# Block edges of an attention, MLP and expert kernel: evictions at the end of a slot, staging in a block's first slot, embeddings fetched sooner, and the second tile's rows turned amid products

## The chip, the cores and the metric

The kernel runs on one core of one Trainium2 chip. The metric is the device time of one execution in microseconds. Three executions of the kernel before took 914.99 to 915.56 us, with a median of 915.32 us.

## What is computed

Three stages follow each other, all in float32 at the interface:

```
attention: q, k, v of (4 batches, 8 heads, 576, 64), causal, window of 128, ALiBi bias
mlp:       h = x @ w_in (512 -> 2048);  g = h * clip(h + 3, 0, 6) / 6;  x = g @ w_out     (2304 rows)
router:    logits = norm(x) @ norm(expert_emb).T / tau;  expert = argmax;  gate = softmax at argmax
experts:   out[rows of e] = gate * (relu(x @ w1[e]) @ w2[e])      (8 experts, 512 -> 1024 -> 512)
```

## The kernel before

Every large product is taken in three passes of a rounded type (fp32r): each operand is split in a high part and a low part (the difference), and high by high, low by high and high by low are summed in PSUM. So between two products there is always a pair of small steps: one engine casts the high part, another subtracts it.

**Attention and MLP run interleaved.** Attention is cut in 40 steps (20 groups of query rows by 2 halves of the heads). One iteration `it` of a loop, written once for each engine, holds `scores(it)`, the softmax of it on DVE and ACT, `transposes(it-1)`, `values(it-2)` and `stage(it+1)`, the transposes that bring q and k of the next step in place (`ps_stage`, copied by ACT in `stage_copy`). The MLP is cut in 9 blocks of 256 rows, and each block in 16 slots, one for each 128 columns of its hidden size: slot m has `up(m)` (12 products of 256 columns into `ps_h`, L736) and, two slots later (LAG = 2), `down(m-2)` (6 products of 512 columns into `ps_y`, L751). Between them ACT makes `clip` (L1027), DVE `gated` (L1247), ACT casts `gated_hi` (L1031), and DVE subtracts `gated_lo` (L1250). `slots(it)` says which slots iteration `it` holds, mostly 3 or 4. The first two of an iteration stand before its transposes, the others behind; on ACT the first two stand between the pairs of exponentials. Iteration 14 has one slot alone (31), iteration 15 begins block 2 with slot 32.

**The block edge.** `ps_y`, two banks of block sums, is emptied once a block: ACT copies bank 0 (L1021) and DVE bank 1 (L1243) to `y_sb`. `down` of the next block's first slot waits for both. In the code before, each engine does so at the start of `slot(m)` with f = LAG, that is slot 2 of the next block:

```
def slot(m):
    blk, f = divmod(m, FC)
    if f == LAG and blk:
        act.wait_ge(pe_g, m - LAG)
        ...
        act.copy(y[:, 0, :], ps_y[0][:]).then_inc(ev_y[0], 1)
```

SP then stores the rows (L417). A block's first `up` waits for `x_lo` of the block's last attention step (L1218), which comes behind that step's `values` (L717), ACT's `x_hi` (L1007) and whatever stands ahead of it in DVE's queue. The blocks' edges lie in iterations 10, 15, 19, 23/24, 28, 33, 37 and 41; in 5, 15, 19, 28, 33 and 37 the iteration's first slot is a block's first.

**The router.** For blocks 0 to 6, DVE takes the dot products of the rows with the 8 unit embeddings (`router`, L1229, 16 instructions a block), spread over the slots of the next block. The embeddings are normalised, written to DRAM and read back to all partitions (`en_all`, 2 MB, L481) by SP at iteration EN_AT, after POOL has split all MLP weights, since they share memory with the weights' staging. Within block 1 the router's instructions stand in slots 25 to 31, two or three in each.

**The expert part.** Rows are gathered by POOL in 25 tiles of 128 rows (`fetch`, L592), turned (`turn_x`, L835), multiplied by w1 (`up_high`, `up_low`, L867), passed through a ReLU by ACT (L1125), turned (`turn_h`, L891), copied by ACT as high part and as raw values (`take_hT`, L1140, L1143), subtracted on POOL (`split_h`, L604; `split_x`, L598, for the tile's rows), multiplied by w2 (`expert_down`, L902) into one bank, and evicted by ACT with the gate as scale (`take_rows`, L1134). POOL scatters them (`put`, L613). `expert_down` has 16 products with the high part, then 8 with the low part; an optional `between` stands between these. The first two tiles (AHEAD) are worked before the tables of all tiles are there, in an order written out by hand: down(0), turn_h(1), down(1). DVE splits the expert weights (L1553, L1555); those of the second expert's w2 wait for `split_h(1)`.

Of the kernel before, what the change touches and what calls it, by code (L numbers as in the profile page):

```python
# [54 lines left out]
def _program(nc, q, k, v, w_in, w_out, emb, tau, w1, w2, y_dram, en_dram, out):  # L55
# [22 lines left out]
    STEPS = NG * NQ  # L78
# [23 lines left out]
    LAG = 2  # L102
# [42 lines left out]
    EMB_AT, EN_AT = FIRST + 2, FIRST + 5  # L145
# [27 lines left out]
    with ExitStack() as ctx:  # L173
# [334 lines left out]
        def _(pool):  # L508
# [122 lines left out]
            fetch(2)  # L631
            fetch(3)
            pool.wait_ge(dve_sc, 3)
            put(0)
            split_h(1)
# [16 lines left out]
        def _(pe):  # L652
# [186 lines left out]
            for it in range(LASTK + 1):  # L839
# [3 lines left out]
                if it < STEPS:  # L843
                    scores(it)
                for m in mine[:2]:
                    slot(m)
# [7 lines left out]
                if it + 1 < STEPS and it >= FIRST:  # L854
                    stage(it + 1)
# [39 lines left out]
            def expert_down(t, between=None):  # L895
# [10 lines left out]
                pe.wait_ge(act_hh, HB * (t + 1))  # L906
                for f in range(FCE):
                    if f % FP == 0:
                        wait(pe, w2_split, NC * e + (f // FP + 1))
# [35 lines left out]
            expert_down(0)  # L945
            turn_h(1)
# [16 lines left out]
        def _(act):  # L963
# [46 lines left out]
            def slot(m):  # L1010
                blk, f = divmod(m, FC)
                if f == LAG and blk:
                    act.wait_ge(pe_g, m - LAG)

                    reach(act, st_y, 16 * (blk - 1))
                    reach(act, dve_dot, 2 * E * min(blk - 1, NBLK - 2))
                    if blk == NBLK:
                        act.wait_ge(pe_yT, 2)
                    if blk == 1:
                        act.wait_ge(st_zero, 16)  # L1020
                    act.copy(y[:, 0, :], ps_y[0][:]).then_inc(ev_y[0], 1)  # L1021
# [22 lines left out]
                if 10 <= f <= FC + 1:  # L1044
                    if f == FC + 1:
                        take_xT(0)
                    first_expert(f - 10)

# [66 lines left out]
            slot(SLOTS + LAG)  # L1115
# [33 lines left out]
            relu(1)  # L1149
            take_rows(0)  # L1150
            take_hT(1)
# [15 lines left out]
        def _(dve):  # L1167
# [65 lines left out]
            def slot(m):  # L1233
                blk, f = divmod(m, FC)
                if f == LAG and blk:
                    dve.wait_ge(pe_g, m - LAG)
                    reach(dve, st_y, 16 * (blk - 1))
                    reach(dve, act_sq, 2 * (blk - 1))
                    if blk == NBLK:
                        dve.wait_ge(pe_yT, 2)  # L1240
                    if blk == 1:
                        dve.wait_ge(st_zero, 16)
                    dve.tensor_copy(y[:, 1, :], ps_y[1][:]).then_inc(ev_y[1], 1)  # L1243
# [7 lines left out]
                if 0 < blk < NBLK - 1 and f > LAG:  # L1251

                    late, span = (6, FC - LAG - 7) if blk == 1 else (0, FC - LAG - 1)
# [37 lines left out]
                if f == FC - 3:  # L1291
                    order_of_experts()

# [201 lines left out]
            slot(SLOTS + LAG)  # L1495
# [100 lines left out]
```

## Time and profile before

| | |
|---|---|
| median of 3 executions | 915.32 us |
| the profiled execution | 914.71 us |
| its span, first to last instruction | 912.7 us |
| TensorE busy | 873.6 us, 96% |
| DVE, ACT, POOL busy | 485.1, 430.3, 234.9 us |
| granted TensorE clock, mean | 0.994 |
| first expert product | at 589 us |

The profile is one execution of the program. Its page gives each engine's busy time, the costliest groups of instructions by line, and the idle time just before them with what ended it. The timeline lists instructions in order of time. "PE" is TensorE's products, "PEld" its weight loads. The ends of products are modelled: two that follow each other without a pause overlap in the record. What lies around the span, 2.0 us of the profiled time, is not in the trace.

### The profile page before, as it was taken

The numbers are of one execution on the slowest core, as the hardware profiler recorded it, in microseconds if no ns is written. First come the engines' busy times: TensorE is split into PE (matmuls) and PEld (weight loads), VectorE is DVE, ScalarE is ACT, GpSimd is POOL, SyncE is SP. The second block draws the span as 40 slices with busy tenths as digits, with TensorE's granted clock in tenths as the row PEclk, the third lists the DMA queues.
The fourth block names the chain that finished last, engine by engine and source line by source line (L and its number), as shares of the span: only waits on it lengthen the run. The fifth ranks groups of instructions, "written<-read, shape, count | busy, mean of one in ns | idle before, by whom it ended". The sixth has DMA issues, their size and how long they took to land.

```text
span 912.7 us, 17359 instructions
## 1 busy us (share of the span) xinstructions
PE 873.6 (96%) x5796; PEld 744.1 (82%) x5796; DVE 485.1 (53%) x1421; ACT 430.3 (47%) x1164; POOL 234.9 (26%) x250
## 2 busy tenths in 40 slices
PE   5799999899999999999999999999999999999996
PEld 4687888788888888888888888877888888888885
DVE  6554447566566565665565656875543454345100
ACT  4667554545544545555545433653334433433441
POOL 6554000000000000000000010237665566556532
PEclk9999999999999999999999999999999999999999
DMA  8453411101111112112100001556554445443100
GB/s 208 115 152 88 145 30 36 47 19 31 41 35 36 41 25 47 36 25 59 24 8 24 2 24 55 156 186 205 158 177 143 139 146 172 159 131 104 40 23 10
DMA packets 84054, 75.38 MB, mean 83 GB/s; under 512 B 62376, under 2 KB 62376, under 8 KB 83842
## 3 DMA queue, kind: packets, MB, share of 16 engines
q1 hardware_dynamic: 78850, 61.81, 23.9%
q0 software_dynamic: 4000, 11.29, 3.7%
q10 hardware_dynamic: 1120, 1.18, 0.4%
q8 instruction: 50, 0.82, 0.4%
q14 instruction: 34, 0.28, 0.1%
HBM read 64.80 MB, written 11.30 MB: 83 GB/s over the span
## 4 chain that ended last, share of the span: by engine, by line
PE 80%; ACT 8%; DVE 7%; issue 3%; DMA 1%; POOL 0%; ACTq 0%; DVEq 0%; POOLq 0%
PE ps_h L736 18%; PE ps_y L751 18%; PE ps_s L902 15%; PE ps_h L867 15%; PE ps_out L717 3%; PE ps_s L685 3%; ACT arena L981 2%; PE ps_y L891 2%; PE ps_s L702 2%; PE ps_stage L666 1%; DVE arena L1203 1%; DVE dot_junk L1229 1%; DVE gated L1247 1%; PE ps_out L835 1%; ACT gated_hi L1031 1%
## 5 line engine op out<-in xcount | busy, mean ns | idle before, releaser
L736 PE MATMUL ps_h<-x_hi,win_hi 128*128 128x256 f32 x576 | 170.7, 296 | 2.3 <-DVE x_lo L1218 2.0
L736 PE MATMUL ps_h<-x_hi,win_lo 128*128 128x256 f32 x576 | 163.2, 283 | 0.0
L736 PE MATMUL ps_h<-x_lo,win_hi 128*128 128x256 f32 x576 | 163.2, 283 | 0.0
L981 ACT ACTIVATE arena<-arena,neg_max 128x256 f32<-128x256 f32 (+3 forms) x160 | 75.7, 475 | 99.9 <-DVE neg_max L1188 99.9
L751 PE MATMUL ps_y<-wout_hi,gated_hi 128*128 128x512 f32 x288 | 115.2, 400 | 5.0 <-ACT y_sb L1021 3.5
L736 PEld LDWEIGHTS ps_h<-x_hi,win_hi 128*128 128x128 f32 x576 | 110.0, 191 | 10.9 <-DVE x_lo L1218 2.9
L1247 DVE SCALAR_TENSOR_TENSOR gated<-clip,ps_h 128x256 f32<-128x256 f32 x144 | 60.4, 420 | 106.3 <-ACT clip L1027 105.9
L1250 DVE TENSOR_TENSOR gated_lo<-gated,gated_hi 128x256 fp32r<-128x256 f32 x144 | 61.9, 430 | 102.3 <-ACT gated_hi L1031 102.3
L1031 ACT CAST gated_hi<-gated 128x256 fp32r<-128x256 f32 x144 | 58.5, 406 | 119.6 <-PE ps_y L751 71.0
L751 PE MATMUL ps_y<-wout_hi,gated_lo 128*128 128x512 f32 x288 | 114.0, 396 | 0.0
L558 POOL MEMSET arena<- 128x64 bf16 x2 | 0.2, 151 | 437.0 <-DVE x_lo L1218 437.0
L751 PE MATMUL ps_y<-wout_lo,gated_hi 128*128 128x512 f32 x288 | 112.4, 390 | 0.0
L736 PEld LDWEIGHTS ps_h<-x_lo,win_hi 128*128 128x128 f32 x576 | 110.3, 191 | 2.4
L736 PEld LDWEIGHTS ps_h<-x_hi,win_lo 128*128 128x128 f32 x576 | 110.2, 191 | 0.0
L1027 ACT ACTIVATE clip<-ps_h,half 128x256 f32<-128x256 f32 x144 | 67.4, 468 | 43.3 <-PE ps_h L736 42.8
L902 PE MATMUL ps_s<-wout_hi,x_hi 128*128 (+1 forms) x200 | 80.2, 401 | 2.9 <-issue 1.9
L1229 DVE CUSTOM_DVE_ANT_0 dot_junk<-y_sb,en_all 128x512 bf16<-128x512 f32 x112 | 76.9, 687 | 4.0
L902 PE MATMUL ps_s<-wout_lo,x_hi 128*128 (+1 forms) x200 | 78.1, 390 | 0.0
L604 POOL TENSOR_TENSOR x_lo<-en_all,x_hi 128x512 fp32r<-128x512 f32 x50 | 59.9, 1216 | 44.6 <-ACT en_all L1143 44.5
L1125 ACT ACTIVATE en_all<-ps_h 128x512 f32<-128x512 f32 x50 | 27.2, 597 | 91.3 <-PE ps_h L867 87.6
L751 PEld LDWEIGHTS ps_y<-wout_hi,gated_hi 128*128 128x128 f32 x288 | 54.9, 191 | 13.4 <-ACT y_sb L1021 4.7
L867 PE MATMUL ps_h<-win_hi,x_hi 128*128 (+1 forms) x200 | 64.3, 402 | 0.5 <-issue 0.4
(215 smaller groups left out, 1645.1 us busy)
## 6 DMA issues: line engine op xcount, KB each, us to landing
arena<-in_moe_w SPq DMA_DIRECT2D x64, 512.0 KB
y_scratch<-y_sb SPq DMA_DIRECT2D x9, 512.0 KB, 4.0
arena<-in_v SPq DMA_DIRECT2D x16, 256.0 KB, 3.0
en_all<-in_moe_w_out SPq DMA_DIRECT2D x16, 256.0 KB, 2.7
arena<-in_q SPq DMA_DIRECT2D x31, 128.0 KB, 2.4
arena<-in_k SPq DMA_DIRECT2D x31, 128.0 KB, 2.8
en_all<-in_moe_w_in SPq DMA_DIRECT2D x12, 256.0 KB, 3.1
en_all<-en_scratch SPq DMA_DIRECT2D x1, 2048.0 KB, 8.2
```

Of the source, the lines that this page charges most:

```text
L604: pool.tensor_tensor(hl[t % 2][:, s], hr[:, s], hh[t % 2][:, s], ALU.subtract).then_inc(pool_hl, 1)
L685: last = pe.matmul(ps_s[hh][0:R, (2 * j + c) * P:(2 * j + c) * P + n], qkT[d, 2 * NP + j, 0:R], qkT[d, 2 * (2 * q4 + j) + c, 0:n], start=T ...
L736: last = pe.matmul(ps_h[m % 2][:, 0:TB], a[:, c, w], r[:, c, x], start=n == 0, stop=n == 3 * KC - 1)
L751: last = pe.matmul(ps_y[t][:], a[f % 2][:, t * P:(t + 1) * P], w[:, f, :], start=f == 0 and n == 0, stop=f == FC - 1 and n == 2)
L867: ins = pe.matmul(ps_hid[b][:], a[:, c * P:(c + 1) * P], w[:, c, bass.ds(e % 2 * FE + b * 512, 512)], start=first, stop=last)
L902: return pe.matmul(ps_out[:], a[:, f * P:(f + 1) * P], w[:, bass.ds(e % 2 * FCE + f, 1), :].rearrange("p a n -> p (a n)"), start=first, st ...
L981: act.activation(a, a, ACT.Exp, bias=nmax[0:R, s % 2, n:n + 1], scale=-1.0, accum_out=rsum[0:R, s % 2, n:n + 1]).then_inc(act_e, 1)
L1027: act.activation(clip[:], ps_h[m % 2][:, 0:TB], ACT.Relu, bias=half[:], scale=1.0 / 6.0).then_inc(act_c, 1)
L1031: act.copy(gh[m % 2][:], gate[:]).then_inc(act_gh, 1)
L1229: dve.tensor_tensor_reduce(out=dot_junk[:], in0=y[:, t, :], in1=en[:, e, :], scale=1.0, scalar=0.0, op0=ALU.mult, op1=ALU.add, accum_out=d ...
L1247: dve.scalar_tensor_tensor(out=gate[:], in0=clip[:], scalar=1.0, in1=ps_h[m % 2][:, 0:TB], op0=ALU.min, op1=ALU.mult).then_inc(dve_g, 1)
L1250: dve.tensor_tensor(gl[m % 2][:], gate[:], gh[m % 2][:], ALU.subtract).then_inc(dve_gl, 1)
```

## The change

Six edits (numbers in code count from 0: tile 1 is the second tile). On ACT and DVE the eviction leaves the start of slot 2 and stands at the end of slot 1 of the next block, as a function of its own with the same waits. TensorE's `stage(it + 1)` goes, in iterations that begin with a block's first slot, from behind the transposes to ahead of the slots. EN_AT is one iteration less, and the first block's router starts in slot 21. `expert_down` waits for the high part in two halves. `turn_h(1)` stands between the high and the low products of tile 0. ACT takes the second tile's turned rows before it evicts tile 0, and POOL splits them before the gather of tile 3.

```diff
-    EMB_AT, EN_AT = FIRST + 2, FIRST + 5
+    EMB_AT, EN_AT = FIRST + 2, FIRST + 4
...
@@ POOL, first two tiles @@
             fetch(2)
+            split_h(1)
             fetch(3)
             pool.wait_ge(dve_sc, 3)
             put(0)
-            split_h(1)
             split_x(2)
...
@@ TensorE, loop over iterations @@
+                stage_first = len(mine) > 0 and mine[0] % FC == 0 and it >= FIRST and it + 1 < STEPS
+                if stage_first:
+
+                    stage(it + 1)
                 for m in mine[:2]:
                     slot(m)
...
-                if it + 1 < STEPS and it >= FIRST:
+                if it + 1 < STEPS and it >= FIRST and not stage_first:
                     stage(it + 1)
...
@@ TensorE, expert_down @@
-                pe.wait_ge(act_hh, HB * (t + 1))
                 for f in range(FCE):
+                    if f % 4 == 0:
+                        pe.wait_ge(act_hh, HB * t + f // 4 + 1)
...
-            expert_down(0)
-            turn_h(1)
+            expert_down(0, between=lambda: turn_h(1))
             expert_down(1, between=lambda: turn_x(2))
...
@@ ACT, and in the same way DVE @@
             def slot(m):
                 blk, f = divmod(m, FC)
-                if f == LAG and blk:
-                    act.wait_ge(pe_g, m - LAG)
...
-                    act.copy(y[:, 0, :], ps_y[0][:]).then_inc(ev_y[0], 1)
...
+                if m >= FC and m % FC == LAG - 1:
+                    evict(m // FC)
+
+            def evict(blk):
+
+                act.wait_ge(pe_g, FC * blk)
+
+                reach(act, st_y, 16 * (blk - 1))
+                reach(act, dve_dot, 2 * E * min(blk - 1, NBLK - 2))
+                if blk == NBLK:
+                    act.wait_ge(pe_yT, 2)
+                if blk == 1:
+                    act.wait_ge(st_zero, 16)
+                act.copy(y[:, 0, :], ps_y[0][:]).then_inc(ev_y[0], 1)
...
-            slot(SLOTS + LAG)
...
             take_hT(0)
             relu(1)
+            take_hT(1)
             take_rows(0)
-            take_hT(1)
             take_xT(2)
...
@@ DVE, router in slots of blocks 1 to 7 @@
-                    late, span = (6, FC - LAG - 7) if blk == 1 else (0, FC - LAG - 1)
+                    late, span = (2, FC - LAG - 3) if blk == 1 else (0, FC - LAG - 1)
```

## Rows read from the trace of the kernel before

**Rows 1.** The page, parts 1 and 5: all engines, and the first down product
```profile
PE 873.6 (96%) x5796; PEld 744.1 (82%) x5796; DVE 485.1 (53%) x1421; ACT 430.3 (47%) x1164; POOL 234.9 (26%) x250
...
L751 PE MATMUL ps_y<-wout_hi,gated_hi 128*128 128x512 f32 x288 | 115.2, 400 | 5.0 <-ACT y_sb L1021 3.5
```

**Rows 2.** Timeline at block edges: start, length, engine, line, [idle before <-releaser]
```profile
109.42 0.50 PE L751 MATMUL ps_y<-wout_hi,gated_hi 128*128 128x512 f32 x1 [0.68 <-ACT y_sb L1021]
...
176.03 0.50 PE L751 MATMUL ps_y<-wout_hi,gated_hi 128*128 128x512 f32 x1 [0.35 <-ACT y_sb L1021]
...
295.67 0.28 PE L736 MATMUL ps_h<-x_lo,win_hi 128*128 128x256 f32 x1
295.79 0.28 PE L736 MATMUL ps_h<-x_hi,win_lo 128*128 128x256 f32 x1
...
297.77 0.47 PE L751 MATMUL ps_y<-wout_hi,gated_hi 128*128 128x512 f32 x1 [1.70 <-ACT y_sb L1021]
...
359.58 0.50 PE L751 MATMUL ps_y<-wout_hi,gated_hi 128*128 128x512 f32 x1 [0.47 <-ACT y_sb L1021]
...
482.07 0.50 PE L751 MATMUL ps_y<-wout_hi,gated_hi 128*128 128x512 f32 x1
```

**Rows 3.** Timeline at the edges at 109 and 297 us: evictions and neighbours
```profile
108.50 0.68 DVE L1243 COPY y_sb<-ps_y 128x512 f32<-128x512 f32 x1
108.81 0.56 ACT L1021 COPY y_sb<-ps_y 128x512 f32<-128x512 f32 x1
...
292.86 0.42 DVE L1250 TENSOR_TENSOR gated_lo<-gated,gated_hi 128x256 fp32r<-128x256 f32 x1 [0.84 <-ACT gated_hi L1031]
...
296.98 0.69 DVE L1243 COPY y_sb<-ps_y 128x512 f32<-128x512 f32 x1
...
302.06 1.03 PE L702 MATMUL ps_s<-ident,arena 128*128 128x128 f32 x8
```

**Rows 4.** Timeline, TensorE at first up products, and four staging transposes
```profile
228.22 0.39 PE L736 MATMUL ps_h<-x_hi,win_hi 128*128 128x256 f32 x1 [1.16 <-DVE x_lo L1218]
...
234.67 0.66 PE L666 MATMUL ps_stage<-ident,arena 128*128 128x128 f32 x4
...
412.10 0.19 PEld L736 LDWEIGHTS ps_h<-x_hi,win_hi 128*128 128x128 f32 x1 [0.32 <-DVE x_lo L1218]
...
473.29 0.39 PE L736 MATMUL ps_h<-x_hi,win_hi 128*128 128x256 f32 x1 [0.88 <-DVE x_lo L1218]
```

**Rows 5.** Timeline, 100 to 165 us: embeddings' copy, routers, iteration 14
```profile
100.89 0.41 SPq L481 DMA_DIRECT2D en_all<-en_scratch  x1
...
156.79 0.68 DVE L1229 CUSTOM_DVE_ANT_0 dot_junk<-y_sb,en_all 128x512 bf16<-128x512 f32 x1
...
157.62 0.69 DVE L1229 CUSTOM_DVE_ANT_0 dot_junk<-y_sb,en_all 128x512 bf16<-128x512 f32 x1
...
158.24 0.48 DVE L1218 TENSOR_TENSOR x_lo<-ps_out,x_hi 128x128 fp32r<-128x128 f32 x2
...
161.71 1.07 PE L702 MATMUL ps_s<-ident,arena 128*128 128x128 f32 x8 [1.77 <-DVE neg_max L1188]
...
164.91 1.09 PE L717 MATMUL ps_out<-arena 128*64 128x128 f32 x16 [1.69 <-ACT arena L993]
```

**Rows 6.** Timeline, second tile's turn, and the last pair of tiles
```profile
612.50 1.03 PE L891 MATMUL ps_y<-ident,en_all 128*128 128x128 f32 x8
...
615.43 0.47 PE L902 MATMUL ps_s<-wout_hi,x_hi 128*128 128x512 f32 x1 [1.89 <-issue]
...
899.74 0.69 ACT L1134 ACTIVATE y_sb<-ps_s,arena 128x512 f32<-128x512 f32 x1 [0.23 <-PE ps_s L902]
...
900.74 0.49 PE L902 MATMUL ps_s<-wout_hi,x_hi 128*128 x1 [1.03 <-ACT y_sb L1134]
```

**Rows 7.** POOL: line L604 (min/median/max ns), and timeline row of a later split
```profile
L604 POOL TENSOR_TENSOR x_lo<-en_all,x_hi x50: 1082/1093/1627, 603.0 to 899.7; 128x512 fp32r<-128x512 f32 x50
...
621.06 1.36 POOL L598 TENSOR_TENSOR x_lo<-en_all,x_hi 128x512 fp32r<-128x512 f32 x1 [0.32 <-ACT en_all L1057]
```

More of the change, by code:

```diff
@@ L1011, in slot @@
                 blk, f = divmod(m, FC)
-                if f == LAG and blk:
-                    act.wait_ge(pe_g, m - LAG)
[L1015 to L1020, printed above, removed]
-                    act.copy(y[:, 0, :], ps_y[0][:]).then_inc(ev_y[0], 1)
                 if m < SLOTS:
@@ L1234, in slot @@
                 blk, f = divmod(m, FC)
[L1235 to L1243, printed above, removed]
                 if m < SLOTS:
@@ L1292, in slot, with evict @@
                     order_of_experts()
+                if m >= FC and m % FC == LAG - 1:
+                    evict(m // FC)
+            def evict(blk):
+                dve.wait_ge(pe_g, FC * blk)
+                reach(dve, st_y, 16 * (blk - 1))
+                reach(dve, act_sq, 2 * (blk - 1))
+                if blk == NBLK:
+                    dve.wait_ge(pe_yT, 2)
+                if blk == 1:
+                    dve.wait_ge(st_zero, 16)
+                dve.tensor_copy(y[:, 1, :], ps_y[1][:]).then_inc(ev_y[1], 1)
             def take_yT(n):
@@ L1494, in _ @@
                     slot(m)
-            slot(SLOTS + LAG)
             first_low(2 * NC - 2)
```

## The prediction

> **What bounds the kernel now.** I read the page first: TensorE is busy 96% of the span [rows 1], so only what stands in TensorE's own queue can move the time. I then asked for TensorE's idle time by line: the first down product of a block waits 5.0 us in all, 3.5 of them for ACT's eviction of the block sums [rows 1]. Third I read the timeline at every block edge, at every block's first up product and at the start of the expert part, and noted each place where two products of one kind start further apart than 0.12 us (up, [rows 2]: 295.67 to 295.79). The reader should see there that TensorE is nowhere short of operands except at such edges, and that in the expert part, once the third tile has begun, products follow each other up to the last pair of tiles. A stall that goes is therefore worth its full length, if the two engines behind it have slack.
>
> **Evictions at the end of their slot.** Nothing is added or removed: each of 8 evictions on ACT and on DVE moves from just before slot 2 of the next block to just after slot 1. What lay between, at the iteration's turn, is softmax work. The wait for the last down product costs nothing in the new place: the fp32r copy just ahead of it in ACT's slot already waits for the same product, and DVE's subtract waits for that copy.
> - Edge at 109 us. DVE's part does not move (it stands right behind the subtract already) and ends at 108.50 + 0.68 = 109.18 [rows 3]. ACT's ended at 109.37 and the product began 0.05 later [rows 2, 3]. New start 109.23 against 109.42: gain 0.19.
> - Edges at 176, 421 (the same 0.35 of idle), 360 and 298 us. The idle printed is 0.35, 0.35, 0.47 and 1.70 [rows 2]; it counts from a modelled end 0.28 after the last start where the next start would come 0.12 after, so 0.16 more is lost each time: 0.51, 0.51, 0.63, 1.86. At 298 us both engines put the softmax of an iteration ahead of the eviction; DVE's subtract ends at 292.86 + 0.42, so the eviction can run to 294.0, two microseconds before the up products end (295.79) [rows 2, 3]. At 482 us no idle is printed, 0.16 is lost [rows 2]. The edge at 236 us has no stall.
> - The eighth edge (the 1.5 us left of the 5.0, [rows 1]) stays: there DVE's cumulative sums stand ahead of the eviction in slot 1 itself. The last eviction keeps its place in order.
> Sum 0.19 + 2 x 0.51 + 0.63 + 1.86 + 0.16 = 3.86 us. What is pushed back: on ACT the copies of turned probabilities and of staged q and k, by up to 0.6 us; on DVE at the 298 us edge the normalisation and scores, by up to 0.69 [rows 3]. They are covered: these scores are done at about 297, and the transposes that wait for them start at 302.06 [rows 3], 300.2 when the stall is gone. From clip on, the order's sum is the same as before.
>
> **Staging in a block's first slot** (6 iterations). Four transposes move from behind the block's first two slots to ahead of its first up product, where TensorE waits for x_lo. Idle before the product is 1.16 us at 228 and 0.88 at 473; at 412 only the weight load shows 0.32 [rows 4], and since a load's idle begins before the product's I count 0.2 of it. The other three iterations have none. Four transposes take 0.66 by their modelled end [rows 4], and eight take 1.03 [rows 6], so four more cost 0.37; bounds 0.37 and 0.66, I take 0.4, nearest to the difference since it is the pitch that moves the next start. Gain 0.4 + 0.4 + 0.2 = 1.0. The q and k pieces were loaded over an iteration before; SP's next load may start earlier, which nobody waits for. In the first such iteration the following wait is ACT's (weight casts), so nothing is gained or lost.
>
> **Embeddings sooner, routers spread.** SP issues the 2 MB copy one iteration earlier: at about 92 us behind a load of v instead of 100.89 [rows 5]. It also waits for POOL's last split of the block weights, which is over by then. The loads of q and k behind it wait for TensorE's staging anyway, and the copy is down long before slot 21; cost nothing. The 16 router products of the first block now spread over 11 slots (21 to 31) instead of 7 (25 to 31), so slot 30 holds one instead of two. That is where it counts: iteration 14 has one slot between scores and transposes, and TensorE idles 1.77 and 1.69 us [rows 5] on a DVE and ACT chain that begins with x_lo at 158.24, right behind two routers. They start 0.83 apart (156.79, 157.62) [rows 5]; with one gone, the whole chain, down to the values at 164.91, comes 0.83 earlier. Gain 0.83. The added routers lie in slots 21 to 24: two of them (1.7 us) now stand ahead of iteration 12's scores, whose transposes come two slots later (5.7 us of products): cost nothing; with that cover gone it would be up to 1.7.
>
> **Second tile's turn amid products.** Eight transposes go between the high and the low products of the first tile, and ACT copies them while TensorE runs on. Now the turn stands last (612.50, 1.03 long) and TensorE waits 1.89 before the next products [rows 6]. Afterwards the low products are last, ending at the same 613.53, and what is then late is ACT's scaled eviction of the single output bank, formerly hidden under the turn. The last pair of tiles already has this very order: the eviction takes 0.69 and the idle is 1.03 [rows 6]. Gain 1.89 - 1.03 = 0.86. Its bounds are 0.86 and 1.1 (these tiles wait on constants, the last pair on registers); I take 0.86. On POOL the second tile's split goes ahead of a gather and comes 6 us sooner (the turn is at about 610.6); the gather and the scatter behind it come up to 3 us later, and the third tile's split, which ran at 621.06 [rows 7], stays within 0.3 us of where it was, 2 us ahead of its products. The extra wait in the middle of each of 25 tiles' high products is met long before; I price it at 0. Not shown alone in the trace, its bound is the start after a wait, 0.50 against a mean of 0.40 [rows 1, 2], 0.1 x 25 = 2.5 us; below zero there is no reason. Nothing around the other waits in these products shows a bubble, so I take 0.
>
> The sum: 3.86 + 1.0 + 0.83 + 0.86 = 6.55 us. The profiled execution took 914.71 us, so 908.2; the median shown is 0.61 above it (915.32), so **908.8 us**.
>
> **Rivals.** About 0.2% (1.8 us) is what a measurement of this kernel can tell from no change.
> - *The edges' gain comes back on ACT.* The eviction, 0.56 to 0.61 us, now precedes pT and staging copies; if TensorE, being sooner, runs into clip or values at six edges, 6 x 0.6 = 3.6 return: 912.4. For it: ACT's idle ahead of the eviction is small at edges. Against it: clip comes no later than now, and its product is read two slots on. Chance 0.17.
> - *POOL becomes late at the start of the experts.* The second tile's split now runs beside DVE's weight splits. Its halves take 1.09 by the median and 1.63 at most [rows 7], a later split 1.36 beside DVE [rows 7], so two halves and the gather, scatter and split behind them could add about 3 us, against 2 us of slack: 1 to 1.5 back, 910.1. The Trainium skill speaks for this (SBUF — State Buffer, section "Who interferes with whom"): the port pair that DVE shares with GpSimd is an exclusive lock, taken against a GpSimd read by a DVE instruction with two SBUF inputs. By that rule each POOL subtract could wait out a DVE subtract, and this rival would hold rather than the forecast; the trace has it in part (1.63 against 1.09). Chance 0.12.
> - *Slower: the softmax ends up behind the eviction.* If an eviction makes scores or turned probabilities late for their transposes, TensorE stalls as it does at 161.71 and 164.91, 3.46 us an edge [rows 5]. Two edges of seven (6.9) decide it, from the point where scores come over 3.1 us later (297.1 to 300.2); all six with softmax between give 908.8 + 20.8 = 929.6. Against: the eviction is only 0.69 long. Chance 0.03.
> - *The change at edges does little* because another wait (x_lo, gated_lo) ends just behind; then only the last two parts and half of the first stay, about 3.6: 911.7. Chance 0.06.
> The forecast keeps 0.62. By itself it spans 907.4 (stage at 0.66 twice, 1.1 in the experts, some spread) to 910.0. The range over all cases is **907.2 to 912.2**. Faster by over 0.2% holds the forecast, the second and fourth and most of the first: 0.91; within 0.2%: 0.06; slower: 0.03.
>
> **What would show it.** In the new profile ACT's and DVE's evictions should start within 0.1 us of the end of their slot's last instruction; the idle before the first down product should fall from 5.0 to about 2 (the eighth edge's 1.5, and 0.5 at 109 us). The up products at 228 and 473 us keep about 0.75 and 0.45 of idle. The waits at 161.71 and 164.91 fall by 0.83 together at the second. The second tile's high products should begin about 1.03 after the low ones end and be released by ACT's scaled eviction. POOL's third split should still end before its products. It is wrong if new idle stands before transposes or values in the iterations after an edge, if DVE's scores in slots 24 to 26 release TensorE, or if products in the middle of a tile start over 0.23 apart.

## The result, and the profile after

The changed kernel takes **904.66 us** (median of 4 executions, 903.44 to 906.94) against 915.31 us (4 executions, 914.99 to 915.56): a ratio of 0.9893, with an interval of 0.9877 to 0.9908. The forecast was 908.8 us, the range 907.2 to 912.2. So the direction was right, and the gain was larger than the whole range allowed. The profiled execution took 906.94 us, the slowest of its four, with a span of 905.0.

The page of the kernel after, in the same two places as [rows 1]:

```profile
PE 870.1 (96%) x5796; PEld 742.4 (82%) x5796; DVE 489.5 (54%) x1421; ACT 430.2 (48%) x1164; POOL 234.2 (26%) x250
...
L751 PE MATMUL ps_y<-wout_hi,gated_hi 128*128 128x512 f32 x288 | 114.4, 397 | 2.0 <-issue 2.0
```

The first down products wait 2.0 us instead of 5.0, as forecast, and no longer for ACT. The timeline at the edges, in order: the first edge; the edge of [rows 4] at 228 us and the block edge behind it; the fourth edge with its evictions; the eighth.

```profile
110.92 0.47 PE L751 MATMUL ps_y<-wout_hi,gated_hi 128*128 128x512 f32 x1 [0.54 <-issue]
...
227.11 0.39 PE L736 MATMUL ps_h<-x_hi,win_hi 128*128 128x256 f32 x1 [0.57 <-DVE x_lo L1225]
...
291.09 0.58 ACT L1055 COPY y_sb<-ps_y 128x512 f32<-128x512 f32 x1
291.56 0.68 DVE L1302 COPY y_sb<-ps_y 128x512 f32<-128x512 f32 x1
...
294.15 0.28 PE L736 MATMUL ps_h<-x_hi,win_lo 128*128 128x256 f32 x1
294.27 0.40 PE L751 MATMUL ps_y<-wout_hi,gated_hi 128*128 128x512 f32 x1
...
533.06 0.47 PE L751 MATMUL ps_y<-wout_hi,gated_hi 128*128 128x512 f32 x1 [1.47 <-issue]
```

The reader is to see at 291 us that both evictions are over by 292.24, two microseconds before the first down product at 294.27, which now follows the last up product by 0.12 us; in [rows 2] it came 1.98 behind it. The first edge keeps its 0.5 and the eighth its 1.5, as foretold. The up product at 227.11 keeps 0.57 of idle and the one that was at 473 keeps 0.65, where about 0.75 and 0.45 were foretold. Iteration 14, which answers to [rows 5]:

```profile
152.96 0.42 DVE L1245 SCALAR_TENSOR_TENSOR gated<-clip,ps_h 128x256 f32<-128x256 f32 x1 [0.32 <-ACT clip L1021]
...
157.14 0.68 DVE L1236 CUSTOM_DVE_ANT_0 dot_junk<-y_sb,en_all 128x512 bf16<-128x512 f32 x1
157.81 0.49 DVE L1225 TENSOR_TENSOR x_lo<-ps_out,x_hi 128x128 fp32r<-128x128 f32 x2
...
161.28 1.07 PE L702 MATMUL ps_s<-ident,arena 128*128 128x128 f32 x8
...
164.48 1.09 PE L717 MATMUL ps_out<-arena 128*64 128x128 f32 x16 [1.70 <-ACT arena L997]
```

Here is the first surprise: I forecast that 0.83 of the 1.77 us ahead of the transposes would go, and all of it went. The values behind keep their 1.70. The two tiles at the start of the expert part, which answer to [rows 6]:

```profile
604.38 1.03 PE L895 MATMUL ps_y<-ident,en_all 128*128 128x128 f32 x8
605.17 2.09 PE L906 MATMUL ps_s<-wout_hi,x_lo 128*128 128x512 f32 x8
606.18 2.83 POOL L604 TENSOR_TENSOR x_lo<-en_all,x_hi 128x512 fp32r<-128x512 f32 x2 [0.56 <-ACT en_all L1150]
607.29 0.69 ACT L1141 ACTIVATE y_sb<-ps_s,arena 128x512 f32<-128x512 f32 x1 [0.23 <-PE ps_s L906]
608.03 0.50 PE L906 MATMUL ps_s<-wout_hi,x_hi 128*128 128x512 f32 x1 [0.78 <-ACT y_sb L1141]
```

The turn stands amid the products and the scaled eviction is what is late, as forecast, for 0.78 us where I took 1.03.

**Where the time went.** To find a gain of this size beside executions that differ by more than a microsecond, I cut each profiled execution at TensorE instructions that every kernel has, and compared the pieces. The cuts are the first product of slot 16 and of slot 131, and the first down product of the first, second, third and last tile. Three of the cuts, in the timeline of the kernel before:

```profile
99.56 0.36 PE L736 MATMUL ps_h<-x_hi,win_hi 128*128 128x256 f32 x1
...
541.73 0.36 PE L736 MATMUL ps_h<-x_hi,win_hi 128*128 128x256 f32 x1
...
606.89 0.50 PE L902 MATMUL ps_s<-wout_hi,x_hi 128*128 128x512 f32 x1
```

and of the kernel after:

```profile
101.19 0.36 PE L736 MATMUL ps_h<-x_hi,win_hi 128*128 128x256 f32 x1
...
535.69 0.36 PE L736 MATMUL ps_h<-x_hi,win_hi 128*128 128x256 f32 x1
...
600.57 0.50 PE L906 MATMUL ps_s<-wout_hi,x_hi 128*128 128x512 f32 x1
```

| piece, us | before, 3 executions | after, 4 executions |
|---|---|---|
| start to slot 16 | 99.48 to 100.00 | 99.47 to 101.19 |
| slot 16 to slot 131 | 442.12 to 442.17 | 434.47 to 434.51 |
| slot 131 to first tile's down products | 63.41 to 65.16 | 63.34 to 64.92 |
| first to second tile's | 8.54 | 7.46 |
| second to third | 20.46 to 21.35 | 20.05 to 20.17 |
| third to last | 264.80 to 264.84 | 264.80 to 264.84 |

(The executions are those shown, the same two kernels run again as b_again, b_again2, a_same, a_again and a_again2.) The second, fourth and sixth pieces repeat within 0.05 us in all of them. So the gain that belongs to the code can be read to a few hundredths: 442.14 - 434.49 = **7.65** in the blocks, 8.54 - 7.46 = **1.08** between the first two tiles, and 20.48 - 20.10 = **0.4** behind them (20.48 from the 20.46 and 20.50 of two of the executions of before, 20.10 the mean of the four of after; the 21.35 of the third has another cause, told below). Together 9.1 us, where 6.55 were forecast. The first, third and fifth pieces also scatter; what is known of the reason stands at the end of the experiments.

### The profile page after: what moved, and what is told of

Read it like the earlier page. It is cut to its first block, busy times and chain, and to the rows that moved or that the text cites. A ratio compares the mean times of both kernels' runs of the same rounds, so it can differ in the third digit from the quotient of the medians.

```text
span 905.0 us, 17361 instructions
## 1 busy us (share of the span) xinstructions
PE 870.1 (96%) x5796; PEld 742.4 (82%) x5796; DVE 489.5 (54%) x1421; ACT 430.2 (48%) x1164; POOL 234.2 (26%) x250
## 4 chain that ended last, share of the span: by engine, by line
PE 86%; ACT 5%; DVE 5%; issue 2%; DMA 1%; POOL 0%; ACTq 0%; DVEq 0%; POOLq 0%
PE ps_h L736 21%; PE ps_y L751 19%; PE ps_s L906 15%; PE ps_h L871 15%; PE ps_out L717 3%; PE ps_s L685 3%; PE ps_s L702 3%; PE ps_y L895 2%; PE ps_stage L666 2%; ACT arena L985 1%; PE ps_out L835 1%; DVE arena L1210 1%; ACT wout_hi L1028 1%; ACT arena L997 1%; DVE gated L1245 1%
## 5 line engine op out<-in xcount | busy, mean ns | idle before, releaser
L604 POOL TENSOR_TENSOR x_lo<-en_all,x_hi 128x512 fp32r<-128x512 f32 x50 | 61.1, 1240 | 46.2 <-ACT en_all L1150 46.2
L751 PEld LDWEIGHTS ps_y<-wout_lo,gated_hi 128*128 128x128 f32 x288 | 54.1, 188 | 12.4
```

What stands on the lines that cost most here:

```text
L604: pool.tensor_tensor(hl[t % 2][:, s], hr[:, s], hh[t % 2][:, s], ALU.subtract).then_inc(pool_hl, 1)
L751: last = pe.matmul(ps_y[t][:], a[f % 2][:, t * P:(t + 1) * P], w[:, f, :], start=f == 0 and n == 0, stop=f == FC - 1 and n == 2)
```

## The experiments

Each kernel was timed against the kernel before on its own chip (b_again2 and a_again2, one execution each, took 913.36 and 904.97 us). "Blocks" below is the piece from slot 16 to slot 131 of its profiled execution.

| kernel | median (lowest to highest), n | ratio to before, interval | blocks |
|---|---|---|---|
| a_same, the kernel after unaltered | 904.08 (903.05 to 904.35), 4 | 0.9881 (0.9864 to 0.9897) | 434.51 |
| a_again, the same | 904.67 (904.22 to 905.80), 4 | 0.9893 (0.9874 to 0.9913) | 434.47 |
| b_again, the kernel before | 914.32 (913.64 to 916.56), 10 | 1.0002 (0.9993 to 1.0012) | 442.12 |
| b_evict | 909.22 (907.58 to 910.77), 6 | 0.9939 (0.9924 to 0.9954) | 437.69 |
| b_router | 913.49 (911.49 to 914.84), 12 | 0.9983 (0.9970 to 0.9995) | 440.33 |
| b_slot30 | 914.38 (912.37 to 915.02), 10 | 0.9994 (0.9982 to 1.0006) | 441.35 |
| b_slot28 | 912.97 (912.21 to 915.41), 10 | 0.9985 (0.9972 to 0.9998) | 441.04 |
| b_turn | 912.53 (911.25 to 914.54), 12 | 0.9976 (0.9963 to 0.9989) | 442.10 |
| b_copy_sooner | 914.22 (911.92 to 915.30), 12 | 1.0002 (0.9993 to 1.0010) | 442.12 |
| a_no_stage | 905.63 (905.01 to 906.92), 4 | 0.9910 (0.9896 to 0.9924) | 435.77 |
| a_stage_later | 905.46 (903.62 to 907.75), 6 | 0.9903 (0.9886 to 0.9920) | 434.49 |
| a_one_wait | 905.38 (902.58 to 906.69), 4 | 0.9914 (0.9900 to 0.9929) | 434.49 |
| a_edge8 | 903.44 (902.12 to 905.93), 5 | 0.9877 (0.9855 to 0.9900) | 433.49 |
| a_best | 901.84 (901.05 to 902.83), 4 | 0.9873 (0.9858 to 0.9887) | 432.23 |

Kernels named a_ start from the kernel after, those named b_ from the kernel before. The intervals are wide against most terms: a single term of 1 us is 0.1%. Where they can't decide, the pieces do.

### Which part holds the gain

**The kernel after again**, in five rounds, as the measure of what is to be divided.

> The changed kernel once more, unaltered. Its four executions so far spread from 903.4 to 906.9 us, those of the kernel before from 915.0 to 915.6. If the spread belongs to the code (its first 70 us came out 1.6 us later in the profiled execution, and must have come out earlier in the others), the executions spread over 2 us again while those of before stay within 1. If it was chance, they lie within 1 us of each other. Either way 902 to 907 us.

It came to 904.08, with the blocks' piece at 434.51: the gain is real.

**The evictions alone.** The kernel before, with ACT's and DVE's `evict` at the end of slot 1:

```diff
-                if f == LAG and blk:
-                    ...
-                    act.copy(y[:, 0, :], ps_y[0][:]).then_inc(ev_y[0], 1)
...
+                if m >= FC and m % FC == LAG - 1:
+                    evict(m // FC)
```

> The kernel before with the evictions at the end of slot 1 alone. By the prediction's term 3.9 us less than before (911.4). By the profile of the changed kernel each edge gave up to 0.1 more than that term, and one of 236 us gave 0.1: 4.3 us less (911.0). If the evictions also free the engines elsewhere, 5 us or more.

The blocks took 437.69, a gain of **4.45** where 3.86 was the term. Part of the difference is at the edge at 236 us, of which the prediction says that it has no stall, since the timeline prints none. The timeline of the kernel before there:

```profile
236.60 0.19 PEld L751 LDWEIGHTS ps_y<-wout_hi,gated_hi 128*128 128x128 f32 x1
236.60 0.50 PE L751 MATMUL ps_y<-wout_hi,gated_hi 128*128 128x512 f32 x1
236.93 0.40 PE L751 MATMUL ps_y<-wout_hi,gated_lo 128*128 128x512 f32 x1
```

and of the kernel after:

```profile
235.07 0.40 PE L751 MATMUL ps_y<-wout_hi,gated_hi 128*128 128x512 f32 x1
235.31 0.40 PE L751 MATMUL ps_y<-wout_hi,gated_lo 128*128 128x512 f32 x1
```

A product that had to wait takes 0.50 instead of 0.40, and the second one starts 0.33 behind it instead of 0.24. Its weight load waits as well: at 236.60 it starts with the product, while in the kernel after it starts at 234.96, one product ahead. So each start after a wait loses another 0.1 us *behind* the product, besides the 0.16 ahead of it that I had counted. From the starts of the up products of both kernels, the edges from 176 us on each gave 0.07 to 0.13 more than the term said, and the first edge its 0.19. The edge at 236 us alone gave 0.13.

**The routers' spread alone.**

```diff
-                    late, span = (6, FC - LAG - 7) if blk == 1 else (0, FC - LAG - 1)
+                    late, span = (2, FC - LAG - 3) if blk == 1 else (0, FC - LAG - 1)
```

> The kernel before with the first block's router instructions spread over 11 slots, the 2 MB copy still at its old place. Predicted was 0.83 us less. Theory from the changed profile: slot 28's third instruction had already made DVE, and through it ACT's chain, late, so the gain is 1.9 us (913.4), with up(32) 1.9 earlier than in the kernel before. Rival: the earlier copy is needed for that; then this gives 0.8 or less.

The blocks took 440.33: a gain of **1.8** (442.14 - 440.33), twice the term of 0.83. This is the largest miss of the sum. The spread differs in two places that could matter, slot 28 (three routers before, one after) and slot 30 (two before, one after). Only slot 30 had been priced, so two more kernels part them. They name the first block's routers by hand: b_slot30 moves one instruction from slot 30 to slot 24 and leaves three in slot 28, b_slot28 moves two from slot 28 to slot 24 and leaves two in slot 30. The tables are keyed by the slot within the block (slot 28 is 12); b_slot30's stands first, b_slot28's behind it:

```diff
-                    for n in range(max(0, g * 2 * E // span), min(2 * E, (g + 1) * 2 * E // span)):
+                    for n in range(*{8: (0, 1), 9: (1, 3), 10: (3, 5), 11: (5, 7), 12: (7, 10),
+                                     13: (10, 12), 14: (12, 13), 15: (13, 16)}...
...
+                    for n in range(*{8: (0, 2), 9: (2, 4), 10: (4, 6), 11: (6, 8), 12: (8, 9),
+                                     13: (9, 11), 14: (11, 13), 15: (13, 16)}...
```

> The kernel before with one router instruction taken from slot 30 and put in slot 24; slot 28 keeps its three. This is the case that the prediction priced: x_lo of step 12 comes 0.83 us earlier, and so does up(32) against up(24). If slot 28 holds a share of its own, no more than 0.83 is seen here. Rival: slot 30 is all of it, then 1.9. The time is under a microsecond below that of the kernel before either way, and the measurement may not tell it; the two marks in the trace do.

> The kernel before with two router instructions taken from slot 28, which keeps one, and put in slot 24; slot 30 keeps its two. Theory: the gate of slot 29 (gated at 152.77 in the kernel before, 1.3 us after its clip was there) comes 1.3 earlier, ACT's chain behind it too, and up(32) comes 1.0 to 1.1 us earlier against up(24). With 0.83 for slot 30 that makes the 1.87 measured for the whole. Rival (slot 30 alone counts): nothing changes at up(32).

Slot 30's instruction is worth 442.14 - 441.35 = **0.79**, as priced. Slot 28's two are worth 442.14 - 441.04 = **1.10**, and the two add up to the spread's 1.8 to 1.9. The timeline of b_slot30, transposes of iteration 14:

```profile
161.12 1.07 PE L702 MATMUL ps_s<-ident,arena 128*128 128x128 f32 x8 [0.95 <-DVE neg_max L1188]
```

and of b_slot28:

```profile
161.99 1.06 PE L702 MATMUL ps_s<-ident,arena 128*128 128x128 f32 x8 [0.67 <-DVE neg_max L1188]
```

Against 1.77 in [rows 5], slot 30 takes 0.82 off the same wait, slot 28 1.10, and both together all that is left. How slot 28 gets there is to be read in the timeline of the kernel before, 6 us ahead of the rows that the prediction looked at:

```profile
150.47 0.68 DVE L1229 CUSTOM_DVE_ANT_0 dot_junk<-y_sb,en_all 128x512 bf16<-128x512 f32 x1
151.00 0.46 ACT L1027 ACTIVATE clip<-ps_h,half 128x256 f32<-128x256 f32 x1
...
152.15 0.69 DVE L1229 CUSTOM_DVE_ANT_0 dot_junk<-y_sb,en_all 128x512 bf16<-128x512 f32 x1
152.77 0.42 DVE L1247 SCALAR_TENSOR_TENSOR gated<-clip,ps_h 128x256 f32<-128x256 f32 x1
153.22 0.41 ACT L1031 CAST gated_hi<-gated 128x256 fp32r<-128x256 f32 x1 [1.77 <-DVE gated L1247]
...
156.32 0.43 ACT L1007 CAST x_hi<-ps_out 128x128 fp32r<-128x128 f32 x2
```

and in that of b_slot28, whose slot 16 begins at 100.93:

```profile
152.88 0.42 DVE L1247 SCALAR_TENSOR_TENSOR gated<-clip,ps_h 128x256 f32<-128x256 f32 x1 [0.32 <-ACT clip L1027]
```

ACT's clip of slot 29 is done at 151.46, but DVE is inside slot 28's three routers until 152.84 and makes `gated` only then; ACT waits 1.77 us for it. `x_hi` is not what holds `x_lo`: ACT is done with it at 156.32 + 0.43 = 156.75, 1.5 us before `x_lo` starts at 158.24 [rows 5]. DVE's own queue holds it. From 152.77 to 158.24 DVE stands idle only twice, 0.47 us each, and both times for ACT's cast of the `gated` that DVE has just made. So the whole queue behind slot 28's routers, with the routers of slots 29 and 30 in it, moves as one piece. In b_slot28, counted from slot 16, `gated` comes at 152.88 - 100.93 = 51.95 us instead of 152.77 - 99.56 = 53.21: 1.26 earlier and not the 1.68 that two routers take, since it is now ACT's clip that it waits for, 0.32 us. `x_lo` comes 1.09 earlier, and the transposes 1.10. In the kernel after, `gated` comes at 152.96 - 101.19 = 51.8. What I had looked at was only the two routers that stand directly ahead of `x_lo`.

**The copy of the embeddings sooner, alone.**

```diff
-    EMB_AT, EN_AT = FIRST + 2, FIRST + 5
+    EMB_AT, EN_AT = FIRST + 2, FIRST + 4
```

> The kernel before with only the 2 MB copy of the embeddings one iteration earlier. Predicted worth 0. Every mark of TensorE from slot 16 to slot 131 lies where it lies in the kernel before, against up(16); time within 0.5 us of it. It also gives one more record of where the granted clock falls in a kernel with the old orders: a stretch at half clock near 550 us or near 612 us is likely.

The ratio is 1.0002 (0.9993 to 1.0010) and the blocks' piece 442.12: worth nothing, as priced. It only makes room for the routers in slot 21.

**The staging.** The kernel after with `stage_first = False`:

> The changed kernel with staging behind the transposes everywhere, as before. Predicted worth was 1.0 us; the sum of the eviction alone (4.45) and the router alone (1.87) leaves 1.3 of what the changed kernel shows up to slot 115, so up(115) is 1.3 later here against up(16), in the iterations with slots 32, 48, 96 and 112. Time 905.4 against 904.1.

The blocks took 435.77, so the new place is worth 435.77 - 434.49 = **1.28** against a term of 1.0. By place, from the starts of the up products of both kernels, it is 0.39 at slot 48 (the place at 228 us in [rows 4]), 0.22 at slot 96 (412 us), 0.57 at slot 112 (473 us), 0.07 at slot 32, and next to nothing at slot 80. The kernel's fifth piece came out 0.7 longer as well. Its timeline shows where: the rows of a later tile landed a quarter of a microsecond late for their turn, and the first product behind the turn (at 628.15) shows another 0.39 of idle, put down to issue.

```profile
627.11 0.42 PEld L835 LDWEIGHTS ps_out<-ident,en_all 128*128 128x128 f32 x4 [0.25 <-DMA en_all<-y_scratch,gather_ids]
```

Nothing in the expert part differs between the two codes, and one execution doesn't say whether this comes back. It shows how little slack the gathers have there, which is the POOL rival's ground.

The staging moved in the first of the six iterations was thought to be worth nothing, since ACT's casts bound there. To see it, the kernel after with `it > FIRST` in place of `it >= FIRST`:

> Staging goes ahead in five iterations, not in the first one with MLP slots (iteration 5). Theory 1: that one move changes the first 70 us, by the order in which TensorE feeds ACT while ACT also casts weights; then the spread goes, and the time is 905.5 to 906.5, with up(8) where it was in the kernel before. Rival: the first 70 us vary for another reason; then it is as the changed kernel, spread and all, within 0.5 us by the median.

From slot 16 on it is the same kernel (434.49), and ahead of it 100.74 lies inside the scatter of 99.5 to 101.2. That place can't be told from nothing.

**The second tile's turn alone**, the kernel before with the three moves of `turn_h(1)`, `take_hT(1)` and `split_h(1)`:

```diff
-            expert_down(0)
-            turn_h(1)
+            expert_down(0, between=lambda: turn_h(1))
```

> The kernel before with the second tile's turn between tile 0's products, and ACT's and POOL's order to it, one wait as before. Predicted was 0.86 us; the changed profile shows 1.08 from down(0) to down(1) and 0.33 more to down(2). Theory: 1.08 comes from the wait being on constants and 0.3 from POOL's split no longer being waited for; so up to 1.4 us less, with the second edit (half waits) no part of it. Also: of the executions with this order the one with the old order alone had a stretch of half clock at 611 us (granted 0.5, next to the idle of 2 us); with the order changed none is expected there. Time 913.2 against 914.7.

The fourth piece fell from 8.54 to 7.46, the whole **1.08** of the kernel after, where the term was 0.86; the fifth came to 20.02 against 20.46 to 20.50. Its timeline shows the same releaser as [rows 6] for the last pair, and less idle:

```profile
613.74 0.50 PE L902 MATMUL ps_s<-wout_hi,x_hi 128*128 128x512 f32 x1 [0.78 <-ACT y_sb L1133]
```

What the fifth piece gained is to be read in the timeline of the kernel before, at the second tile's low products. They need the halves that POOL splits:

```profile
618.59 2.15 POOL L604 TENSOR_TENSOR x_lo<-en_all,x_hi 128x512 fp32r<-128x512 f32 x2
619.74 2.24 PE L902 MATMUL ps_s<-wout_hi,x_lo 128*128 128x512 f32 x8
620.79 0.76 PEld L902 LDWEIGHTS ps_s<-wout_hi,x_lo 128*128 128x128 f32 x4 [0.28 <-POOL x_lo L604]
```

POOL's first half is done at 619.69, and the first low product starts at 619.74; the second half is done at 620.74, and the fifth starts at 620.79. So the old order made TensorE wait twice for `split_h(1)`. In b_turn the split stands earlier, is over at 614.73, and the low products start at 617.88. From the start of the second tile's products to the end of its low ones (the start of the next tile's first product) the kernel before takes 6.60 us and b_turn 6.07: that is where the 0.4 comes from, with a little lost again behind.

**The half waits.** The kernel after with the old single wait ahead of the loop:

```diff
+                pe.wait_ge(act_hh, HB * (t + 1))
                 for f in range(FCE):
-                    if f % 4 == 0:
-                        pe.wait_ge(act_hh, HB * t + f // 4 + 1)
```

> The changed kernel with the single wait for both halves of the turned rows ahead of a tile's high products. Predicted worth of the half waits, for good or bad: 0, bound 2.5 us. If the extra wait cost anything, the 22 tiles between the third and the last would each be shorter here than 12.27 us; if the half wait let the second tile start sooner, down(1) would be later here. I expect neither, and no difference in time (within 0.5 us).

Every piece that repeats is the same within a few hundredths (434.49, 7.47, 264.8): worth 0 in either direction. The bound of 2.5 us that I had set fell. A wait that is met when it is reached does not show in the products.

### What is left at the edges, and a faster version

At the eighth edge DVE's cumulative sums of the router's choice stand ahead of its eviction in slot 1. Taking DVE's eviction ahead of them there is one line:

```diff
+                    evict(m // FC)
                     sum_up()
...
-                if m >= FC and m % FC == LAG - 1:
+                if m >= FC and m % FC == LAG - 1 and m != LAST + 1:
```

> The changed kernel, with DVE's eviction at the eighth edge also ahead of the cumulative sums (it stood behind them). The idle of 1.47 us before the first down product of the last block goes; the sums are 0.7 us later, and prefix(0), two slots on, can take that. Gain 1.6 us against the changed kernel. If a stretch of half clock at 543 to 550 us is provoked by that idle, it goes too, and up to 1.5 more is won in the executions that have it: 901.5 to 903. Rival: prefix(0) waits for the late sums instead; then under 0.5.

The blocks' piece fell by 1.0 where I expected 1.6 (903.44 in all). The timeline of a_edge8:

```profile
531.43 0.68 DVE L1303 COPY y_sb<-ps_y 128x512 f32<-128x512 f32 x1
532.22 0.47 PE L751 MATMUL ps_y<-wout_hi,gated_hi 128*128 128x512 f32 x1 [0.44 <-issue]
```

0.44 is left: the eviction ends at 532.11, right behind the slot's subtract, and in front of both DVE has been busy without a break since 527.94 with `choose` and `gated`, but for the 0.47 us of the cast.

**Both remaining levers together.** If slot 28 taught the right thing, the other blocks' routers in their last slot should cost something too. a_best is a_edge8 with the span of blocks 2 to 7 one slot shorter:

```diff
-                    late, span = ... else (0, FC - LAG - 1)
+                    late, span = ... else (0, FC - LAG - 2)
```

> The changed kernel with DVE's eviction ahead of the sums at the eighth edge, and the router instructions of blocks 1 to 6 done by slot 14 of the next block, so that none stands ahead of x_lo at a block's end. The waits of 0.74 and 0.76 us before up(48) and up(112), which DVE's two routers and the copy of their sums make, go, and 0.2 at up(96): 1.7 us less than the run with the eighth edge alone, 2.7 less than the changed kernel, some 901.5. Rival: x_hi is as late as x_lo at those edges; then 0.5 or less beyond the eighth edge's 1.0.

It takes **901.84** (901.05 to 902.83), 0.9873 of the kernel before (0.9858 to 0.9887). By the blocks' piece it beats the kernel after, 432.23 against 434.49; the two were not timed side by side on one chip, and the intervals of their ratios overlap. The gain was a little smaller than expected, 2.3 us of the blocks' piece for 2.7: two edges gave 0.83 and 0.73, but one wait, ahead of slot 96, grew by 0.6. In the kernel after:

```profile
405.90 0.66 PE L717 MATMUL ps_out<-arena 128*64 128x128 f32 x8 [0.30 <-ACT arena L1000]
```

and in a_best:

```profile
403.63 0.66 PE L717 MATMUL ps_out<-arena 128*64 128x128 f32 x8 [0.92 <-ACT arena L1000]
```

### The rest of the measured difference

The code gives 9.1 us by the pieces that repeat, while the medians differ by 10.65 in the first measurement, 10.6 for a_same and, in the last, 914.39 - 904.67 = 9.7. The two kernels were run again to see how often each piece takes which value.

> The kernel before, unaltered, for a second record of it. Theory: three stretches vary from execution to execution in either kernel (up to slot 16; slots 131 on to the first expert product, where the granted clock falls for some microseconds in some executions; and, in the old order only, the start of the second tile), the rest repeats within 0.1 us. So up(16) to up(131) takes 442.2 us again, and the clock falls near 550 us, near 613 us, at both or at neither.

> The same once more, one execution: again 442.2 us from up(16) to up(131), and the other stretches as they fall. If the old order of the second tile invites the fall of the clock at its idle of 2 us, some of these records show half clock there.

> The changed kernel, unaltered. From up(16) to up(131) 434.5 us (7.67 less than before) and 1.08 less again from down(0) to down(1) of the experts; no fall of the clock near 606 us. The median difference to the kernel before is 9.1 from these parts and 0.5 to 1.5 from falls of the clock that it has less often: 10 to 10.6.

> The same once more, one execution: the fixed parts as above; near 544 us the clock falls or not. If it fell in every record of the changed kernel, a chance in the fall there would be ruled out; two of the changed kernel so far show one each way.

What moves the third and fifth pieces is TensorE's granted clock. The view by stretches (length, then busy time of TensorE's products, its loads, DVE, ACT and POOL, then clock, share of DMA and GB/s), of the kernel before:

```profile
546.00:552.00 6.00, 5.59 (x36) 5.02 (x36) 4.12 (x18) 1.79 (x5) 0.00 (x0) 0.86 0.00 0
```

of the kernel after, the profiled execution first shown:

```profile
540.00:546.00 6.00, 5.59 (x34) 5.02 (x33) 4.09 (x18) 1.76 (x5) 0.00 (x0) 0.80 0.00 0
```

and of a_same, the same kernel in another execution:

```profile
538.00:544.00 6.00, 5.59 (x41) 4.98 (x41) 4.46 (x20) 2.28 (x8) 0.00 (x0) 1.00 0.00 0
```

Near 550 us the clock falls for a short stretch from 2.4 to 1.2 GHz in some executions of both kernels, which lengthens the third piece from between 63.2 and 63.9 us to between 64.6 and 65.2, about 1.4. The products are busy 5.59 of the 6 us both where it falls and where it doesn't. Among what TensorE does ahead of it are 16 products of only 8 columns, behind a short idle, in the kernel before at

```profile
548.02 1.92 PE L803 MATMUL ps_out<-embeddings_T,arena 128*128 128x8 f32 x16 [0.41 <-DVE arena L1296]
```

These products stand in all 18 profiled executions, so they alone don't bring the fall. It is no part of the change, but whether it comes is part of an execution's time. It did in 9 of 18 profiled executions, on both sides. The second place is the turn of the second tile. Of b_again and b_again2, the kernel before twice:

```profile
612.00:618.00 6.00, 4.35 (x12) 3.48 (x13) 2.78 (x3) 1.55 (x4) 5.09 (x5) 0.72 0.77 260
```

```profile
612.00:618.00 6.00, 4.11 (x21) 3.21 (x19) 3.21 (x4) 2.02 (x5) 4.72 (x4) 1.00 0.94 289
```

and of a_again, the kernel after:

```profile
605.00:611.00 6.00, 5.34 (x25) 4.42 (x26) 5.90 (x6) 1.50 (x4) 5.21 (x5) 1.00 0.75 250
```

With the old order TensorE idles 1.89 us there [rows 6]; in 4 of the 8 profiled executions with that order the clock fell right behind it and the fifth piece was 21.35 instead of 20.5. In none of the 10 with the new order did it fall there. By these counts the change is worth another 0.45 us on average (half of 0.9), which makes 9.6 of the 9.7 to 10.65 measured. That is a count of 18 executions, not a proof that the shorter idle keeps the clock; what is left, up to 1 us, lies within the scatter of the first 100 us (98.6 to 101.4 over all kernels), of the place near 550 us, and of chips. That remains open. The clock falls in the first 50 us too, in 16 of the 18, but the two without a fall there took 99.3 and 101.4, so it does not explain the scatter of that piece by itself.

## Why the prediction was wrong in size

- **What bounds the kernel**, and that a stall that goes is worth its full length: right. Nothing of the edges' gain came back in the blocks.
- **Evictions**: the mechanism was right, edge by edge; 4.45 instead of 3.86. The term left out what a wait costs behind the first product.
- **Staging**: 1.28 instead of 1.0, inside what the bounds of its four transposes allow; the first iteration can't be told from 0. Why slot 112 gave 0.57 and slot 48 only 0.39 is not shown.
- **Copy of the embeddings**: 0, as priced.
- **Router spread, the step that failed.** The prediction said "slot 30 holds one instead of two. That is where it counts", and took 0.83. That instruction is worth 0.79; slot 28's two are worth 1.10 more. The step looked back from `x_lo` only as far as the two routers directly ahead of it. DVE's queue had no slack of its own from slot 28's routers on, 6 us before the rows that were read.
- **Second tile's turn**: right in mechanism, 1.08 instead of 0.86. The upper bound of 1.1 was the right one to take; whether constants instead of registers are the reason, no run separates.
- **POOL's earlier split, a second step that failed.** The prediction moved `split_h(1)` 6 us forward and put its gain at nothing. TensorE had waited for both of its halves in the old order, which is 0.4. In the same step the third tile's split was to stay "within 0.3 us of where it was, 2 us ahead of its products". Counted from the second tile's first product it came at 616.62 - 608.03 = 8.59 us instead of 621.06 - 615.43 = 5.63, and TensorE now waits for it (below).
- **Half waits**: 0, as priced.

Summed: 0.98 (the routers' 1.81 less 0.83) + 0.59 + 0.28 + 0.22 + 0.4 = 2.5 us more than 6.55, so all five misses lie on the same side. The blocks gained 7.65 in all, 0.1 more than the three parts measured alone. Where a term had two bounds I had mostly taken the lower value. From 908.8 that gives 906.3, already outside the range; the clock and the scatter make up the rest to 904.7. The lower end of the range was built from the bounds of the terms alone. It held nothing for the scatter of executions, though the kernel before ranged over 3 us on one chip (912.16 to 915.20 in 17 executions beside a_best) and over 5.5 on another (912.43 to 917.95 in 29 beside b_turn); the three shown at first lay within 0.6 by luck.

**The rivals.** *The gain comes back on ACT* did not: pT, values and staging behind the evictions bring no new wait of TensorE's in the blocks. *The softmax behind the eviction* neither. *The edges do little* is refuted by b_evict. *POOL late at the experts* did not hold by its price, 1 to 1.5 us back, but it came near. The two subtracts of `split_h(1)` took 2.83 us in all (shown above), and the third tile's split behind the gather and the scatter is late for its low products:

```profile
616.62 1.10 POOL L598 TENSOR_TENSOR x_lo<-en_all,x_hi 128x512 fp32r<-128x512 f32 x1
617.77 0.99 PEld L871 LDWEIGHTS ps_h<-win_hi,x_lo 128*128 128x128 f32 x5 [0.32 <-POOL x_lo L598]
```

It ends at 617.72, and the first low product starts at 617.77, 0.29 behind the one before, the next 0.34 behind it, where 0.23 is the usual distance: 0.17 us lost, and one of the prediction's signs of being wrong (products over 0.23 apart in the middle of a tile). In the kernel before that split was over 3.4 us ahead of these products (622.42 against 625.79). So the new order has used up POOL's slack, and a split 1 us later would cost 1 us (an estimate). The rule of the Trainium skill that I had named beside it (SBUF — State Buffer, section "Who interferes with whom") is borne out in part: in the same execution, the first tile's two took 2.15 and the one that ran beside DVE's splits 1.54 instead of 1.09.

```profile
596.72 2.15 POOL L604 TENSOR_TENSOR x_lo<-en_all,x_hi 128x512 fp32r<-128x512 f32 x2 [1.40 <-ACT en_all L1150]
...
607.47 1.54 POOL L604 TENSOR_TENSOR x_lo<-en_all,x_hi 128x512 fp32r<-128x512 f32 x1
```

That lengthening stands ahead of the third tile's split in POOL's queue, so part of the 0.17 us may be its; no run separates the two. a_no_stage's gather shows as well how little slack is left.

## What to carry to other kernels

When an operand is late, follow it back through the queue of the engine that makes it, past the short waits for what the other engine hands straight back, to the last wait that this other engine really sets. Every instruction in between delays the operand by its length, even two slots earlier. When an instruction is moved forward, ask whether anyone waited for it in its old place, and what it pushes back in the new one. When a stall goes, count the start after it as well. And where a kernel is full, cut the profiled executions of both versions at common instructions and compare the pieces, since they repeat to hundredths where medians scatter by microseconds; the range of a forecast has to hold that scatter too.

## What was not expected of the hardware

- A product that has waited takes 0.50 us instead of 0.40, and the next starts 0.33 behind it instead of 0.24: a wait is followed by about 0.1 us of loss that no idle column prints (236.60 and 235.07 us above). Its weight load starts with it instead of one product ahead.
- TensorE is granted 1.2 instead of 2.4 GHz for short stretches in a kernel whose products fill 96% of the span. One such place, near 550 us, comes in half of the profiled executions of either kernel, with products busy 5.59 of 6 us in the same stretch where it came and where it did not.
- A semaphore wait that is already met, 25 times amid products, costs nothing that these records show.
